# Loading an expert's weights as four serial quarters from one point in time, and one branch per expert slot instead of two

## The chip, the cores and the metric

The kernel runs on one core of one Trainium2 chip. The metric is the device time of one execution in microseconds, as the median of several runs. Engines are named as in the profile: PE (matrix multiply; PEld its weight loads; PEldq its sequencer), DVE, ACT, POOL and SP, which issues most of the DMAs. Three runs of the kernel before gave 836.25 us as the median.

## The reference

Attention with exponential features, then a gated two-layer network, then a mixture of experts. Cut to the last stage, which the change touches:

```python
def _moe2_ref(x, w_gate, w_output_gate, w1, w2):        # x: 2304 x 512, E = 8, F = 1024
    logits = x @ w_gate
    e_idx = np.argmax(logits, axis=1)                   # one expert for each token
    ...
    for e in range(E):
        mask = e_idx == e
        h = np.maximum(x[mask] @ w1[e], 0.0)            # 512 -> 1024
        ye = h @ w2[e]                                  # 1024 -> 512
        out[mask] = gate_w[mask, None] * eom[mask, e, None] * ye
```

## The kernel before

The kernel has three stages one after the other: attention (to about 183 us), the dense network in six blocks of 384 tokens (to about 572 us), and the experts (from 572 us to 824 us). Float32 products are made of three float16 products each: both factors are split into a high and a low part, and low times low is left out (`PARTS`).

In the second stage DVE and ACT also split the weights of all eight experts, and SP stores them in HBM (`split`): for each expert `e` and each matrix `m` (0 is w1, 1 is w2) two halves, the high parts and the low parts, of 1 MB each. So one expert is four pieces of 1 MB.

The third stage works in slots. A slot is up to 128 tokens of one expert, and there are `SLOTS` = 27 of them. The tokens have been scattered by expert into `rows` in HBM. For each slot: POOL gathers 128 rows into `xg` (L668), PE transposes them (L969, 8 matmuls), DVE copies them to `xgt` (L1695), PE multiplies by w1 (`slot_hidden`, L979, 96 matmuls of 128 columns), ACT makes the high part of the ReLU (L1262) and DVE the low part (L1704), PE multiplies by w2 (`slot_output`, L991, 24 matmuls of 512 columns), DVE scales the result (L1714), and POOL scatters it to `out` (L681).

Slots 0 to 2 (`EARLY`) belong to the expert that the first blocks' tokens chose most, "star"; they are written out straight. Slots 3 to 24 are run by a loop of two slots a turn, slots 25 and 26 by the same function `slot` behind it. Which expert a slot has is known only at run time. DVE makes a table of it (L1738 to L1784), `table_ready` tells that it is there, and for every slot PE reads `slot_code` (L1035): whether the slot is used, the parity of its expert's buffer, and `need`, how far the weights must have landed. A slot that isn't used takes two small matmuls (L1054, L1058) instead of the large ones. The program holds the code of both parities, and branches choose between them at run time.

Weights stand in two buffers, `w1_sb[b]` and `w2_sb[b]`, b = 0, 1. Load number k goes into buffer k % 2: k = 0 is the star expert, k = 1 is expert 0, k = 2 is expert 1, and so on to k = 8. All are issued by SP, in the order of its program, with `load_expert(k, e, a, m, half)` at L510; each raises `ew1_loaded` or `ew2_loaded` by 16 when it has landed. A load must wait until the expert that held the buffer before is done with it: `eh_done` counts halves of the first product, `eo_done` second products, and `free_at[e]` is the number of the slot up to which that holds.

On the DMA engines the expert loads (queue q1) meet POOL's gathers and scatters (q0) and fetches of instructions (q8 and q14).

Of the kernel before, what the change touches and what calls it, by code (L numbers as in the profile page):

```python
# [48 lines left out]
EARLY = 3  # L49
# [26 lines left out]
def moe_program(nc, qkt_in, v, w_phi, w_in, w_out, w_gate, w_ogate, w1, w2, out, rows, split, recs):  # L76
# [8 lines left out]
    with ctx:  # L85
# [285 lines left out]
        def _(sp):  # L371
# [133 lines left out]
            def load_expert(k, e, a, m, half):  # L505

                dst, done = ((w1_sb, ew1_loaded), (w2_sb, ew2_loaded))[m]
                if k and not half:
                    sp.wait_ge(done, 32 * k)
                sp.dma_start(dst[a].rearrange("p l c f -> p (l c f)")[:, half * UW:(half + 1) * UW],  # L510
                             split[bass.ds(e, 1), m, :, half * UW:(half + 1) * UW].rearrange("o p n -> (o p) n")).then_inc(done, 16)
# [10 lines left out]
            for half in range(2):  # L522
                load_expert(1, 0, 1, 1, half)
            sp.wait_ge(eh_done, 2 * EARLY)
            for half in range(2):
                load_expert(2, 1, 0, 0, half)
            sp.wait_ge(eo_done, EARLY)
            for half in range(2):
                load_expert(2, 1, 0, 1, half)

            sp.wait_ge(table_ready, 1)
            for e in range(2, E):
                free = sp.value_load(free_at[0:1, e:e + 1], min_val=EARLY, max_val=EARLY + 2 * MAINS)
                sp.wait_ge(eh_done, free * 2)
                for m in range(2):
                    if m == 1:
                        sp.wait_ge(eo_done, free)
                    for half in range(2):
                        load_expert(e + 1, e, (e + 1) % 2, m, half)
# [179 lines left out]
        def _(pe):  # L719
# [311 lines left out]
            slot_transposes(4, 0, 3)  # L1031

            def slot(s, a, turn, more=True):
                p = s - EARLY
# [5 lines left out]
                with pe.If(used):  # L1040
                    with pe.If(parity):
                        slot_hidden(a, 1)
                    with pe.Else():
                        slot_hidden(a, 0)
                    if more:
                        slot_transposes(s + 2, a, turn)
                    pe.wait_ge(ew2_loaded, need)
                    pe.wait_ge(og_ready, s - 1)
                    with pe.If(parity):
                        slot_output(s, a, 1)  # L1050
                    with pe.Else():
                        slot_output(s, a, 0)
                with pe.Else():
# [785 lines left out]
```

## Time and profile before

| | before |
|---|---|
| median of three runs | 836.25 us (835.92 to 836.63) |
| the profiled execution | 836.25 us, span 834.6 us |
| PE busy | 810.8 us, 97% of the span |
| DVE, ACT, POOL busy | 559.7, 387.0, 180.2 us |
| granted TensorE clock, mean | 0.995 |
| share of PE in the chain that ended last | 78% |
| expert loads (L510) | 36 of 1024 KB |

The span goes from the first to the last instruction; 1.65 us of the profiled execution lie outside it. "Busy" of PE means that a matmul is under way. The chain that ended last is followed back from the last instruction, at each step to what released it. For a small change the places count at which PE is idle, and what would make it idle next.

### The profile page before, as it was taken

The numbers are of one execution on the slowest core, as the hardware profiler recorded it, in microseconds if no ns is written. First come the engines' busy times: TensorE is split into PE (matmuls) and PEld (weight loads), VectorE is DVE, ScalarE is ACT, GpSimd is POOL, SyncE is SP. The second block draws the span as 40 slices with busy tenths as digits, with TensorE's granted clock in tenths as the row PEclk, the third lists the DMA queues.
The fourth block names the chain that finished last, engine by engine and source line by source line (L and its number), as shares of the span: only waits on it lengthen the run. The fifth ranks groups of instructions, "written<-read, shape, count | busy, mean of one in ns | idle before, by whom it ended". The sixth has DMA issues, their size and how long they took to land.

```text
span 834.6 us, 19302 instructions
## 1 busy us (share of the span) xinstructions
PE 810.8 (97%) x7110; PEld 509.6 (61%) x7111; DVE 559.7 (67%) x1119; ACT 387.0 (46%) x841; POOL 180.2 (22%) x211
## 2 busy tenths in 40 slices
PE   7999999999999999999999999999899999999995
PEld 5666666665555555555555555556667777777773
DVE  4778888898888888888898897845622543222221
ACT  5777788883654645645646546534101221101110
POOL 4555556761000010010000001010221322111100
PEclk9999999999999999999999999999999999999998
DMA  7466667856665865865764755483173925256500
GB/s 228 136 196 213 203 189 221 222 177 222 221 212 190 223 244 181 258 213 209 220 253 168 252 218 209 122 340 140 60 284 124 392 76 221 91 228 245 233 27 15
DMA packets 67447, 164.36 MB, mean 197 GB/s; under 512 B 28614, under 2 KB 32966, under 8 KB 60736
## 3 DMA queue, kind: packets, MB, share of 16 engines
q1 hardware_dynamic: 61472, 146.74, 51.8%
q0 software_dynamic: 5760, 16.80, 5.6%
q8 instruction: 36, 0.59, 0.3%
q14 instruction: 19, 0.16, 0.1%
q10 hardware_dynamic: 160, 0.07, 0.0%
HBM read 114.16 MB, written 47.55 MB: 194 GB/s over the span
## 4 chain that ended last, share of the span: by engine, by line
PE 78%; DVE 8%; POOL 5%; ACT 4%; issue 3%; another core or an unknown queue 1%; ACTq 0%; DVEq 0%; POOLq 0%
PE ps L894 19%; PE ps L883 17%; PE ps L991 14%; PE ps L979 13%; POOL arena L591 4%; PE ps L771 3%; PE ps L743 3%; PE ps L799 3%; DVE u_mx L1511 2%; ACT arena L1095 2%; PE ps L757 2%; DVE y_words L1503 1%; DVE arena L1536 1%; PE ps L969 1%; PE ps L808 1%
## 5 line engine op out<-in xcount | busy, mean ns | idle before, releaser
L883 PE MATMUL ps<-arena,w_in_sb 128*128 128x384 f16 x1152 | 200.9, 326 | 0.0
L894 PE MATMUL ps<-w_out_sb,arena 128*128 128x512 f16 x576 | 171.3, 379 | 1.3 <-DVE stage L1597 1.3
L883 PEld LDWEIGHTS ps<-arena,w_in_sb 128*128 128x128 f16 x1152 | 111.9, 98 | 81.1 <-issue 0.2
L1262 ACT ACTIVATE x_t<-ps 128x512 f16<-128x512 f32 x54 | 31.6, 596 | 203.8 <-PE ps L979 173.0
L979 PE MATMUL ps<-x_t,arena 128*128 128x128 f16 x2112 | 121.5, 219 | 1.4 <-issue 1.4
L979 PEld LDWEIGHTS ps<-x_t,arena 128*128 128x128 f16 x2112 | 119.2, 98 | 5.3 <-issue 1.8
L991 PE MATMUL ps<-arena,x_t 128*128 128x512 f16 x528 | 119.7, 383 | 2.4 <-DVE x_t L1704 2.4
L894 PE MATMUL ps<-w_out_sb,stage 128*128 128x512 f16 x288 | 109.1, 379 | 0.0
L1234 ACT ACTIVATE arena<-relu 128x384 f16<-128x384 f32 x96 | 50.0, 520 | 119.0 <-DVE relu L1592 119.0
L894 PEld LDWEIGHTS ps<-w_out_sb,arena 128*128 128x128 f16 x576 | 55.7, 98 | 61.5 <-issue 4.5
L1704 DVE SCALAR_TENSOR_TENSOR x_t<-ps,x_t 128x512 f16<-128x512 f32 x54 | 36.7, 689 | 82.4 <-ACT x_t L1262 82.4
L1095 ACT ACTIVATE arena<-ps,arena 128x128 f32<-128x128 f32 x288 | 79.8, 394 | 26.1 <-DVE arena L1287 17.7
L991 PEld LDWEIGHTS ps<-arena,x_t 128*128 128x128 f16 x528 | 51.0, 99 | 60.5 <-ACT x_t L1262 2.8
L1223 ACT ACTIVATE relu<-ps,three,s_h 128x384 f32<-128x384 f32 x96 | 63.4, 661 | 46.3 <-PE ps L883 46.1
L591 POOL TENSOR_TENSOR arena<-arena 128x512 f32<-128x512 f32 (+1 forms) x64 | 69.5, 1085 | 66.5 <-ACT arena L1095 60.8
L1536 DVE SCALAR_TENSOR_TENSOR arena<-arena,u_up 128x1024 f16<-128x1024 f32 x64 | 79.3, 1280 | 4.7 <-ACT arena L1211 4.7
L1211 ACT ACTIVATE arena<-arena,u_up 128x1024 f16<-128x1024 f32 x64 | 72.5, 1140 | 5.6 <-DVE u_up L1528 5.6
L1511 DVE TENSOR_REDUCE u_mx<-arena 128x1 f32<-128x1024 f32 x64 | 74.8, 1211 | 0.0
L641 POOL PARTITION_ALL_REDUCE u_all<-u_red x16 | 7.8, 488 | 301.3 <-DVE u_red L1515 301.3
L1285 DVE TENSOR_REDUCE arena<-ps 128x8 f32<-128x1024 f32 (+1 forms) x48 | 45.9, 957 | 37.2 <-PE ps L743 37.2
L1592 DVE SCALAR_TENSOR_TENSOR relu<-relu,ps 128x384 f32<-128x384 f32 x96 | 52.7, 549 | 25.5 <-ACT relu L1223 24.1
L1714 DVE TENSOR_SCALAR x_t<-ps,stage 128x512 f32<-128x512 f32 x27 | 20.2, 748 | 69.2 <-PE ps L991 69.2
(201 smaller groups left out, 911.8 us busy)
## 6 DMA issues: line engine op xcount, KB each, us to landing
arena<-split SPq DMA_DIRECT2D x36, 1024.0 KB
arena<-in_moe_w SPq DMA_DIRECT2D x16, 2048.0 KB
split<-arena SPq DMA_DIRECT2D x16, 2048.0 KB, 7.4
arena<-in_qkt SPq DMA_DIRECT2D x15, 576.0 KB, 6.5
stage<-in_moe_w_in SPq DMA_DIRECT2D x16, 512.0 KB, 5.0
stage<-in_moe_w_out SPq DMA_DIRECT2D x16, 512.0 KB, 6.2
x_t<-rows POOLq DMA_DIRECT2D x27, 257.0 KB
y_words<-recs SPq DMA_DIRECT2D x32, 144.0 KB, 3.0
```

The source lines that it names most:

```text
L591: nc.gpsimd.tensor_tensor(out, x, y, ALU.add).then_inc(sum_step, 1)
L883: last = nc.tensor.matmul(ps[:, HB[f % GB], 0:BN], w_in_sb[:, lw, c, f * P:(f + 1) * P], xt[:, a, lx, c, :], start=c == 0 and lw + lx == 0 ...
L894: last = nc.tensor.matmul(ps[:, YB + r, :], g_sb[lg_][:, f % GB, r * P:(r + 1) * P], w_out_sb[:, lw, f, :], start=f == 0 and lg_ + lw == 0 ...
L979: last = nc.tensor.matmul(ps[:, bank, f % 4 * P:(f % 4 + 1) * P], w1_sb[b][:, lw, c, f * P:(f + 1) * P], xgt[:, a, lx, c, :], start=c == 0 ...
L991: last = nc.tensor.matmul(ps[:, 6 + a, :], hg[:, a, lh, f, :], w2_sb[b][:, lw, f, :], start=f == 0 and lh + lw == 0, stop=f == EFC - 1 and ...
L1095: last = nc.scalar.activation(pk[:, t0 + t, s, :], ps[:, bank, t * F:(t + 1) * F], ACT.Exp, bias=bias[:, t0 + t:t0 + t + 1], scale=1.0 - 2 ...
L1211: nc.scalar.activation(split_sb[:, 0, q_ * Q:(q_ + 1) * Q], raw[b][:, q_ * Q:(q_ + 1) * Q], ACT.Copy, scale=u_up[:, b:b + 1]).then_inc(u_h ...
L1223: nc.scalar.activation(relu3[:, f % GB, :], ps[:, HB[f % GB], 0:BN], ACT.Relu, bias=three[:, 0:1], scale=s_h[:, 0:1]).then_inc(relu3_ready, 1)
L1234: nc.scalar.mul(g_sb[0][:, f % GB, :], relu3[:, f % GB, :], CG / 6.0).then_inc(g_hi, 1)
L1511: nc.vector.tensor_reduce(u_mx[:, q_:q_ + 1], raw[b][:, q_ * Q:(q_ + 1) * Q], AX.X, ALU.max, apply_absolute_value=True).then_inc(u_searche ...
L1536: nc.vector.scalar_tensor_tensor(out=split_sb[:, 1, cols], in0=raw[b][:, cols], scalar=u_up[:, b:b + 1], in1=split_sb[:, 0, cols], op0=ALU ...
L1592: nc.vector.scalar_tensor_tensor(out=relu3[:, f % GB, :], in0=relu3[:, f % GB, :], scalar=6.0, in1=ps[:, HB[f % GB], 0:BN], op0=ALU.min, o ...
```

## The change

It does two things.

On SP, the four loads of an expert are ordered and gated in another way. Before, w1's two halves went out one behind the other when the first product of the last slot was done (`eh_done`), and w2's two halves when its second product was done (`eo_done`). Now all four wait for `eo_done`, they alternate (w1 high, w2 high, w1 low, w2 low), and each waits until the piece before it of the same matrix has landed. So at most two are under way, one of each matrix. This holds for the star expert and expert 0 too, except that those keep their order of m and half.

On PE, in `slot`, the branch on the parity is taken once instead of twice. The new function `used_slot` holds the first product, the transposes of slot s + 2, the two waits and the second product, and stands once for each parity. The transposes so stand twice in the program.

```diff
             def load_expert(k, e, a, m, half):
                 dst, done = ((w1_sb, ew1_loaded), (w2_sb, ew2_loaded))[m]
-                if k and not half:
-                    sp.wait_ge(done, 32 * k)
+                if k or half:
+                    sp.wait_ge(done, 32 * k + 16 * half)
                 sp.dma_start(dst[a].rearrange("p l c f -> p (l c f)")[:, half * UW:(half + 1) * UW],
...
-            sp.wait_ge(eh_done, 2 * EARLY)
-            for half in range(2):
-                load_expert(2, 1, 0, 0, half)
             sp.wait_ge(eo_done, EARLY)
             for half in range(2):
-                load_expert(2, 1, 0, 1, half)
+                for m in range(2):
+                    load_expert(2, 1, 0, m, half)
...
-                sp.wait_ge(eh_done, free * 2)
-                for m in range(2):
-                    if m == 1:
-                        sp.wait_ge(eo_done, free)
-                    for half in range(2):
+                sp.wait_ge(eo_done, free)
+                for half in range(2):
+                    for m in range(2):
                         load_expert(e + 1, e, (e + 1) % 2, m, half)
...
+            def used_slot(s, a, turn, more, need, b):
+                slot_hidden(a, b)
+                if more:
+                    slot_transposes(s + 2, a, turn)
+                pe.wait_ge(ew2_loaded, need)
+                pe.wait_ge(og_ready, s - 1)
+                slot_output(s, a, b)
...
                 with pe.If(used):
                     with pe.If(parity):
-                        slot_hidden(a, 1)
+                        used_slot(s, a, turn, more, need, 1)
                     with pe.Else():
-                        slot_hidden(a, 0)
-                    if more:
-                        slot_transposes(s + 2, a, turn)
-                    pe.wait_ge(ew2_loaded, need)
-                    pe.wait_ge(og_ready, s - 1)
-                    with pe.If(parity):
-                        slot_output(s, a, 1)
-                    with pe.Else():
-                        slot_output(s, a, 0)
+                        used_slot(s, a, turn, more, need, 0)
```

How SP's program stands at the loads of experts 1 and 2 (k = 2 and 3), before:

```order
L510 DMA arena<-split 128x4096 [waits ew1_loaded,eh_done]
L510 DMA arena<-split 128x4096
L510 DMA arena<-split 128x4096 [waits ew2_loaded,eo_done]
L510 DMA arena<-split 128x4096
L533 TENSOR_LOAD free_at [waits table_ready]
L533 ISA x2
L534 REGISTER_ALU
L510 DMA arena<-split 128x4096 [waits ew1_loaded,eh_done]
L510 DMA arena<-split 128x4096
```

and with the change:

```order
L510 DMA arena<-split 128x4096 [waits ew1_loaded,eo_done]
L510 DMA arena<-split 128x4096 [waits ew2_loaded]
L510 DMA arena<-split 128x4096 [waits ew1_loaded]
L510 DMA arena<-split 128x4096 [waits ew2_loaded]
L531 TENSOR_LOAD free_at [waits table_ready]
L531 ISA x2
L510 DMA arena<-split 128x4096 [waits ew1_loaded,eo_done]
L510 DMA arena<-split 128x4096 [waits ew2_loaded]
```

The wait for `eh_done` is gone, and every load now waits for a landing.

How PE's program stands at slot 3, the first of the loop, from the branch on the parity, before (first both copies of the first product, then the transposes, then the first copy of the second product):

```order
L1041 COMPARE_AND_BRANCH
L979 MATMUL ps<-x_t,arena 128x128 x96
L1041 UNCONDITIONAL_BRANCH
L979 MATMUL ps<-x_t,arena 128x128 x96
L1043 UNCONDITIONAL_BRANCH
L965 ISA
L969 MATMUL ps<-ident,x_t 128x128 [waits xg_loaded1]
L969 MATMUL ps<-ident,x_t 128x128 x7
L1048 REGISTER_ALU [waits ew2_loaded]
L1049 COMPARE_AND_BRANCH [waits og_ready]
L988 REGISTER_ALU
L991 MATMUL ps<-arena,x_t 128x512 [waits hg_ready,hg_hi]
```

and with the change:

```order
L1045 COMPARE_AND_BRANCH
L975 MATMUL ps<-x_t,arena 128x128 x96
L961 ISA
L965 MATMUL ps<-ident,x_t 128x128 [waits xg_loaded1]
L965 MATMUL ps<-ident,x_t 128x128 x7
L1034 REGISTER_ALU [waits ew2_loaded]
L984 REGISTER_ALU [waits og_ready]
L987 MATMUL ps<-arena,x_t 128x512 [waits hg_ready,hg_hi]
L987 MATMUL ps<-arena,x_t 128x512 x11
L984 REGISTER_ALU
L987 MATMUL ps<-arena,x_t 128x512 [waits hg_ready,hg_hi]
L987 MATMUL ps<-arena,x_t 128x512 x11
```

The second copy of the first product, over which the sequencer jumped in the middle of the slot, now stands behind the whole slot with its own transposes and second product, and is jumped over at the slot's end.

## Rows read from the trace of the kernel before

**Rows 1.** The profile's page: part 1, engines' busy time, and part 3, the instruction fetches.

```profile
PE 810.8 (97%) x7110; PEld 509.6 (61%) x7111; DVE 559.7 (67%) x1119; ACT 387.0 (46%) x841; POOL 180.2 (22%) x211
...
q8 instruction: 36, 0.59, 0.3%
```

**Rows 2.** Timeline of PE, 592 to 601 us: start, us, operation, [idle before it <- releaser].

```profile
596.25 4.44 PE L991 MATMUL ps<-arena,x_t 128*128 128x512 f16 x12 [2.36 <-DVE x_t L1704]
```

**Rows 3.** The chain that ended last, 612 to 630 us: start, us, what.

```profile
612.12 5.36 PE ps L979 x96
617.49 0.45 PE ps L969 x8
617.93 5.18 PE ps L991 x24
623.11 1.36 issue
624.47 5.53 PE ps L979 x96
```

**Rows 4.** The same chain, 655 to 666 us.

```profile
658.72 5.42 PE ps L979 x96
```

**Rows 5.** Branches of PE's sequencer at L1049, whole span; then 618 to 624 us alone.

```profile
L1049 PEldq COMPARE_BRANCH  x30: 69/169/3622, 617.0 to 818.0; - x30
...
L1049 PEldq COMPARE_BRANCH  x1: 3622/3622/3622, 619.1 to 619.1; - x1
```

**Rows 6.** L1041, 616 to 618 and 628 to 630 us; L1049, 628 to 633.

```profile
L1041 PEldq COMPARE_BRANCH  x1: 332/332/332, 616.3 to 616.3; - x1
...
L1041 PEldq COMPARE_BRANCH  x1: 306/306/306, 628.9 to 628.9; - x1
...
L1049 PEldq COMPARE_BRANCH  x2: 69/378/687, 629.4 to 631.6; - x2
```

**Rows 7.** The DMA queue of instructions from 620 to 621, then from 629.5 to 630.5 us.

```profile
q8 instruction: 1, 0.02, 5.8%
...
q8 instruction: 1, 0.02, 6.8%
```

**Rows 8.** DMA queues from 634 to 801 us: every queue that moved something.

```profile
q1 hardware_dynamic: 3456, 25.17, 37.9%
q0 software_dynamic: 3120, 8.38, 14.5%
q14 instruction: 2, 0.02, 0.0%
```

**Rows 9.** Windows: us, busy by engine, PEclk, DMA share, GB/s.

```profile
598.00:600.00 2.00, 2.00 (x6) 0.63 (x5) 1.83 (x9) 0.00 (x0) 0.00 (x0) 0.50 0.00 0
...
610.00:612.00 2.00, 2.00 (x17) 1.17 (x16) 0.29 (x2) 0.00 (x0) 0.55 (x1) 1.00 1.04 438
...
618.00:620.00 2.00, 2.00 (x11) 0.94 (x10) 1.48 (x5) 0.12 (x1) 0.00 (x0) 1.00 0.91 334
620.00:622.00 2.00, 2.00 (x11) 0.91 (x10) 0.00 (x0) 0.00 (x0) 0.55 (x1) 1.00 0.42 117
...
624.00:626.00 2.00, 1.53 (x28) 1.54 (x29) 0.02 (x1) 0.00 (x0) 1.02 (x1) 1.00 0.00 0
```

**Rows 10.** SP's loads at L510, first and last start: 611 to 613, then 646 to 650 us.

```profile
L510 SPq DMA_DIRECT2D arena<-split x2: 328/380/433, 611.7 to 612.1; - x2
...
L510 SPq DMA_DIRECT2D arena<-split x2: 328/381/434, 646.6 to 647.0; - x2
```

**Rows 11.** The same line from 541 to 545, then 551 to 553 us.

```profile
L510 SPq DMA_DIRECT2D arena<-split x4: 333/356/711, 541.8 to 543.4; - x4
...
L510 SPq DMA_DIRECT2D arena<-split x2: 338/412/486, 551.8 to 552.2; - x2
```

**Rows 12.** PE's wait for w1 (L1038) at slot 9; POOL's gathers (L668), 650 to 657 us.

```profile
L1038 PEldq ALU_OP  x1: 36/36/36, 657.8 to 657.8; - x1
...
L668 POOL DMA_DIRECT2D x_t<-rows x2: 552/553/554, 650.1 to 655.4; - x2
```

## The prediction

> **What bounds the kernel now.** I read the page first: PE has a matmul under way for 810.8 of 834.6 us [rows 1]. So I looked for the places from 572 us on where PE is idle, since only the expert stage is touched. The timeline and the chain show two. At 593.9 us PE stands 2.36 us for DVE's L1704, and the twelve matmuls behind it take 4.44 us instead of 2.6 [rows 2]. At 623.11 us it stands 1.36 us, released by "issue": PE waits for no engine, its own sequencer is late [rows 3]. Elsewhere up to 824 us a slot is 5.36 (L979) + 0.45 (L969) + 5.18 (L991) = 10.99 us without a gap [rows 3], and no wait of PE for a weight load is among them. The change can therefore save nothing by loading better. It can touch the 1.36 us, and it can open new gaps.
>
> **Why PE stands at 623.11.** The sequencer runs ahead of the matmuls by what is queued: at 619.1 us it has handed out the whole second product of slot 3, which ends at 623.11, so it has 4.0 us in hand. Then its jump at L1049 takes 3.62 us, where the median of 30 such jumps is 0.17 [rows 5]. So slot 4's code is there at 622.7, and behind its register work the first matmul starts at 624.47 [rows 3], 1.75 us later. The sum is 3.62 + 1.75 - 4.0 = 1.4, the gap. During the jump one packet of q8 runs, from 620 to 621 us [rows 7]; q8 moves 0.59 MB in 36 packets, 16 KB each, of instructions [rows 1]. The next such packet that can be told apart is at 629.5 to 630.5 us; behind it a jump at 631.6 takes 0.69 us [rows 6, 7]. From 634 to 801 us there is none at all, so the loop's code is held once it has been passed [rows 8]. The long jump is a first pass over code that has not arrived.
>
> When was that code asked for? I take it that it is asked for when the sequencer enters the piece before it. In the second case that is the jump in the middle of slot 4, at 628.9 us [rows 6]: the packet starts between 629.5 and 630.5, say 1.0 us later, and the code is there at 631.6 + 0.69 = 632.3, 3.4 us after the request. In the first case it is the jump at L1041 at 616.3, which ends at 616.7 [rows 6]. There the packet starts only between 620 and 621 [rows 7], some 3.5 us later and not 1.0: the DMA engines are full until 620 (share 0.91, then 0.42 [rows 9]) with the loads issued at 606 and 611.7 [rows 10]. So the stall is one instruction fetch that stood behind an expert load.
>
> **Part 1, PE's code.** The change takes away the jump in the middle of the slot, 0.33 us in slot 3 [rows 6]. It lies beside the first product, which the sequencer leads by about 1 us, so it is worth nothing, and so in all 22 slots. The transposes stand twice in the program but run once: nothing. What moves is the place of code. Before, the mid-slot jump over a copy of 96 matmuls brought the sequencer at 616.7 into the next piece and asked for the one after it, 2.4 us before the jump at 619.1. Now the sequencer passes 96 + 8 + 24 matmuls in a row and then makes a single jump at the slot's end over a whole slot's copy. The piece with slot 4's code is asked for in the last instructions of the second product or by the jump itself, at 618.9 to 619.1. If nothing were in the way it would be there 3.4 us later, at 622.4, a gain of 0.3. If it waits as long as the one before (3.5 in place of 1.0) it is there at 625.0, a loss of 2.3.
>
> **Part 2, the loads that meet it.** The four loads of expert 1 now start at 611.7 (before: two at 606.1, two at 611.7 [rows 10]). A load of 1 MB at the 438 GB/s of a full window [rows 9] is 2.4 us. Before, 4 MB and the gathers were through by 620. Now 4 MB that start to move at about 613 and share with one gather and one store end near 625. Thus the fetch that is asked for at 619 falls into a full stretch in any case. At most two loads are queued, so I take a wait of about one of them less what has run, 1.3 us rather than the 2.5 seen before. The code is there at 619.0 + 3.4 + 1.3 = 623.7 us, against 622.7. **Term 1: +1.0 us, ends -0.3 and +2.3.**
>
> The Trainium skill's page "Runtime: NRT & Kernel Launch", section "Instruction fetch mechanics", says that prefetch is sequential and that a taken branch out of a window of two pages forces a fetch. By that rule each slot's long jump would cost a fetch; rows 8, with no q8 packet in 167 us of such jumps, speak against it, and it is a rival below. The page "DMA: Bandwidth & Descriptors", section "Queues, rings and completion order", says that a DMA engine takes turns between queues only at the end of a packet. The late packet of rows 7 agrees; it gives no other sum.
>
> **Part 3, later weights.** Loads of w1 start one second product (5.6 us) later than before, and every piece waits for the last one of its matrix. Each expert with two slots or more hides that: its loads have 22 us. The tight place is expert 2, since expert 1 has only slot 7 (647 to 658). Its w1 loads were issued at 641.0 and are now due at 646.6 [rows 10]. PE asks for them at slot 9, at 657.8 [rows 12], and with an unused slot in front it has next to nothing in hand there: its first matmul of slot 9 starts at 658.72 [rows 4], 0.9 us later, and the register work alone takes most of that. So 11.2 us are left for w1 low, the third of four MB. The nearest row: at 541.8 four loads were issued together, and w1's second, the third MB, had landed at 551.8, 10.0 us later [rows 11]. That is 656.6. Two gathers (650.1 and 655.4 [rows 12]) and one store of 256 KB, 0.6 us each, share the engines: +0.6 to +1.8, so 657.2 to 658.4. The serial issue adds nothing as long as w2 high is still moving when w1 low is issued, and it moves for 2.4 us while an issue takes about 1.1. **Term 2: +0.1 us, ends 0 and +1.0.** w2 is needed 5.5 us later and lands at about 660.5: nothing. Behind these loads SP has only the next expert's to issue, and they all start from `eo_done`.
>
> **Part 4, the first loads.** Star and expert 0 now go out piece by piece from 541.8. Star, issued at 541.8 and landed some 12 us later, is needed at 572; expert 0's last two loads, which wait for the end of the dense stage at 572 as before, are needed behind slot 3's first product, at 617.9 [rows 3]. A few us more are hidden in both. The gathers of slots 0 and 1 are issued at 563 behind the scattered rows, which share with fewer loads than before: nothing.
>
> **The sum** is made against the profiled execution, 836.25 us, which is also the median: 836.25 + 1.0 + 0.1 = 837.35, say 837.4 us.
>
> **The rivals.**
> 1. The fetch finds a gap between two loads, or the shorter burst before 619 leaves it free. Then term 1 is 0 or negative, to the whole 1.36 at most: 834.9 to 836.2. For it: only two loads are queued instead of four. Against it: 4 MB from 613 on can't be over by 619. Chance 0.2.
> 2. The gap at 623 grows past 2 us and PE's clock falls. Rows 2 show it: behind the 2.36 us gap twelve matmuls took 4.44 instead of 2.6, 1.85 us lost, at a granted clock of 0.50, the 1.2 GHz level; behind the 1.36 us gap it stayed at 1.00 [rows 2, 9]. Term 1 is then +1.2 to +2.3 and +1.85 comes on top: 839.3 to 840.5. It decides from a gap of about 2 us. Against it: my middle value for the gap is 2.4 us, just at that edge, and the half of the cases below it stays clear. Chance 0.15, slower.
> 3. w1 of expert 2 lands late, beyond 657.8 by 0.5 to 1.5 us; in sum 838 to 839. Chance 0.15.
> 4. Faster: the gap of 2.36 us at 593.9 and its 1.85 us of slow clock shrink, since ACT, on which DVE waits there, was released by nothing that the profile names. If that is a fetch of ACT's that meets other traffic now, up to 4.2 us go: 832 to 834.5. Nothing that the change moves runs at 590. Chance 0.05.
> 5. By the rule of the Runtime page each of about 20 used slots pays its long jump: 20 gaps of 1.4 us, 864 us. Chance 0.01.
>
> **How the numbers follow.** The forecast's case has 0.44, from 836.0 to 838.7. 0.2% is about what a measurement of this kernel can tell from no change: 1.67 us, the limits are 834.6 and 837.9. Faster holds rival 4 and a little of rival 1: 0.07. Slower holds rivals 2, 3 and 5 and a quarter of the forecast's case: 0.40. The rest, 0.53, is the same. The range from 835.4 to 840.2 leaves out rival 4, the fast end of rival 1 and the last of rival 2.
>
> **What would show it.** The gap before slot 4, 1.36 us now, is 2 to 3 us, with a q8 packet inside the sequencer's long jump, which now stands at the end of slot 3. No gap at slot 9, and SP's third load of expert 2 is issued near 651.5. The mid-slot jump is gone and the slots still take 10.99 us. The prediction is wrong if the gap at 623 vanishes or stays as it is, if PE waits for weights at any other slot, or if PE's gap at 593.9 has changed.

## The result and the profile after

The kernel after took 840.96 us as the median of six runs (839.78 to 843.92), the kernel before 835.48 us beside it (833.18 to 836.63). The ratio is 1.0055, with a 95% interval from 1.0032 to 1.0079: slower by 2.7 to 6.6 us. The record holds 31 more executions of the kernel after: over all 37 the median is 839.78 us (835.77 to 844.21). The forecast was 837.4 us with a range up to 840.2. The median of the 37 lies inside it and that of the six 0.8 us outside. The sign was right, but the forecast called a change within 0.2% the likeliest, and its added time of 1.1 us is a quarter to a fifth of what was measured.

The profiled execution of the kernel after took 835.77 us, span 834.1 us, which is the lowest of the 37. So its rows are read for gaps, and its total is not taken for the kernel's. The page, where rows 1 stood:

```profile
PE 807.9 (97%) x7110; PEld 508.1 (61%) x7111; DVE 559.6 (67%) x1119; ACT 387.0 (46%) x841; POOL 180.1 (22%) x211
...
q8 instruction: 36, 0.59, 0.3%
```

The work is the same, and so is the number of code packets (36). The timeline of PE at the two places where before stood [rows 2, 3], first 588 to 600 us, then 612 to 636:

```profile
590.69 5.34 PE L987 MATMUL ps<-arena,x_t 128*128 128x512 f16 x24
...
621.92 5.53 PE L975 MATMUL ps<-x_t,arena 128*128 128x128 f16 x96 [3.47 <-issue]
...
634.57 1.62 PE L975 MATMUL ps<-x_t,arena 128*128 128x128 f16 x26 [1.49 <-issue]
```

At 593 us there is no gap in this execution: 24 matmuls of L987 (L991 before) run in one piece at full clock. Where before stood 1.36 us ahead of slot 4, PE now stands 3.47 us, and 1.49 us ahead of slot 5, where it did not stand at all before. The chain that ended last shows the third place, slot 9:

```profile
612.96 7.11 DMA arena<-split
620.08 1.85 issue
621.92 5.53 PE ps L975 x96
...
633.08 1.49 issue
...
657.82 0.36 issue
658.18 5.53 PE ps L975 x96
```

The matmuls themselves take what they took in rows 3. The chain puts the first gap down to a weight load that lands at 620.07 us. That is no more than the last semaphore event ahead of the gap; slot 4 uses expert 0, whose weights had long landed, and the experiments come back to it. What PE's sequencer did is in its branches at L1045, the single parity jump of a slot (whole span, then 612 to 618, then 628 to 632 us; ns min/median/max, and when):

```profile
L1045 PEldq COMPARE_BRANCH  x30: 63/177/5773, 606.6 to 811.2; - x30
...
L1045 PEldq COMPARE_BRANCH  x1: 5773/5773/5773, 614.4 to 614.4; - x1
...
L1045 PEldq COMPARE_BRANCH  x1: 3289/3289/3289, 629.0 to 629.0; - x1
```

Two jumps are long, and the median of 30 is 0.18 us. The first starts at 614.42 and ends at 620.19; the first matmul follows 1.73 us later, at 621.92. Slot 3's second product ends at 618.45, so the sequencer had 4.03 us in hand: 5.77 + 1.73 - 4.03 = 3.47, the gap. The code packets of q8 lie inside both jumps, at 617.81 and at 630.02 us (the windows 617 to 618 and 630 to 631):

```profile
q8 instruction: 1, 0.02, 5.8%
...
q8 instruction: 1, 0.02, 6.0%
```

The DMA engines round them (us, busy by engine, PEclk, DMA share, GB/s):

```profile
616.00:618.00 2.00, 2.00 (x11) 0.89 (x10) 0.00 (x0) 0.00 (x0) 0.14 (x1) 1.00 0.99 412
618.00:620.00 2.00, 0.45 (x3) 0.00 (x0) 0.75 (x1) 0.00 (x0) 0.00 (x0) 1.00 1.02 345
620.00:622.00 2.00, 0.08 (x2) 0.09 (x3) 0.00 (x0) 0.00 (x0) 1.02 (x1) 1.00 0.90 328
622.00:624.00 2.00, 2.00 (x38) 2.00 (x39) 0.00 (x0) 0.00 (x0) 0.00 (x0) 1.00 0.56 225
...
628.00:630.00 2.00, 2.00 (x11) 0.93 (x10) 1.48 (x5) 0.09 (x1) 0.00 (x0) 1.00 0.00 0
```

The first jump starts in full traffic, and the packet comes 3.4 us after the jump's start. The second starts in a window with no traffic, and the packet comes after 0.97 us. In both cases the jump ends 2.3 to 2.4 us after the packet's start. Ahead of slot 5 the sequencer also needs more than the 1.73 us: it first closes the loop's turn, which makes 2.23 us from the jump's end at 632.34, and 3.29 + 2.23 - 4.03 = 1.49, the second gap. The burst of weight loads now lasts longer. Against the end of slot 3's second product the last packet of q1 ended 0.8 us ahead before (622.3 against 623.11) and ends 5.9 us behind it now (624.3 against 618.45). SP's loads (L510) of the expert 1, its last two, and of the expert 2, its last two, then SP's wait for w1 of the expert 2 (L509), where rows 10 stood:

```profile
L510 SPq DMA_DIRECT2D arena<-split x2: 328/328/328, 613.0 to 617.2; - x2
...
L510 SPq DMA_DIRECT2D arena<-split x2: 327/328/328, 650.8 to 654.3; - x2
...
L509 SPq EVENT_SEMAPHORE  x1: 17/17/17, 657.4 to 657.4; - x1
```

**The account.** Against the profiled execution of before: +2.11 at slot 4 (3.47 against 1.36), +1.49 at slot 5, +0.36 at slot 9, together +3.96 us, 0.47%. In the other direction the stop at 593.9 and its slow clock are absent, 2.36 and 1.85 us [rows 2], which are 4.21 of the 4.66 us by which slot 3 ends sooner (618.45 against 623.11 [rows 3]): 834.6 + 3.96 - 4.66 is 833.9, and the span is 834.1. (Times of the two traces can therefore only be compared against a slot's own.) The stop at 593 is not the change's doing, as the runs below show, so the change by itself costs about 4 us in this trace, within the interval of the timed runs.

### The profile page after: what moved, and what is told of

It reads as the page before. It is cut to its first block, busy times and chain, and to the rows that moved or that the text cites. A ratio compares the mean times of both kernels' runs of the same rounds, so it can differ in the third digit from the quotient of the medians.

```text
span 834.1 us, 19259 instructions
## 1 busy us (share of the span) xinstructions
PE 807.9 (97%) x7110; PEld 508.1 (61%) x7111; DVE 559.6 (67%) x1119; ACT 387.0 (46%) x841; POOL 180.1 (22%) x211
## 4 chain that ended last, share of the span: by engine, by line
PE 76%; DVE 8%; POOL 5%; ACT 4%; issue 4%; DMA 2%; ACTq 0%; DVEq 0%; POOLq 0%
PE ps L890 19%; PE ps L879 17%; PE ps L987 13%; PE ps L975 13%; POOL arena L587 4%; PE ps L767 3%; PE ps L739 3%; PE ps L795 3%; DVE u_mx L1507 2%; ACT arena L1091 2%; DMA arena<-split 2%; PE ps L753 2%; DVE y_words L1499 1%; DVE arena L1532 1%; PE ps L804 1%
## 5 line engine op out<-in xcount | busy, mean ns | idle before, releaser
L987 PE MATMUL ps<-arena,x_t 128*128 128x512 f16 x528 | 117.9, 379 | 0.0
L1700 DVE SCALAR_TENSOR_TENSOR x_t<-ps,x_t 128x512 f16<-128x512 f32 x54 | 36.7, 689 | 82.4 <-ACT x_t L1258 82.4
L987 PEld LDWEIGHTS ps<-arena,x_t 128*128 128x128 f16 x528 | 50.5, 98 | 56.8
```

Source lines behind the costliest of these rows:

```text
L987: last = nc.tensor.matmul(ps[:, 6 + a, :], hg[:, a, lh, f, :], w2_sb[b][:, lw, f, :], start=f == 0 and lh + lw == 0, stop=f == EFC - 1 and ...
```

## The experiments

Each was timed in rounds against the kernel before on the same chip. The gaps are those of PE in one profiled execution of each. The kernel before itself was profiled only once, so its gap of 1.36 us is taken over to the other chips; the kernels with its branches and with the loads of the change, profiled on two of them, had 1.34 and 1.25 us there. One theory stands behind most of them. **Theory A:** PE's code comes in pieces of 16 KB; a piece is asked for when the sequencer enters the one before it; and a request that falls into a burst of weight loads comes late. The rivals are that the slot waits for weights, that the single branch costs by itself, and that the new waits of SP cost by themselves.

### Each half of the change alone

**One branch alone.** Before's loads, and PE's program as changed:

```diff
                     with pe.If(parity):
-                        slot_hidden(a, 1)
+                        used_slot(s, a, turn, more, need, 1)
                     with pe.Else():
-                        slot_hidden(a, 0)
-                    ...
+                        used_slot(s, a, turn, more, need, 0)
```

> The change's PE part alone (one branch per slot, used_slot); SP loads as before. Theory A (the loss is the code's: code is asked for only when the sequencer gets to the piece before it, and one jump at the slot's end asks too late): both gaps of the changed kernel stay, before slot 4 (1.4 to 3.5 us, by how much of the load burst is left at 618 us) and before slot 5 (about 1.5 us); no gap at slot 9; time +1.5 to +3.6 us over before. Theory B (the loss is the loads': later, serial loads): one gap of 1.36 us before slot 4 as before, none before slot 5, time as before within 0.5 us.

Measured: 833.67 us against 831.82, ratio 1.0016 [1.0003, 1.0029]. Its chain from 614 to 641 us:

```profile
619.96 2.34 issue
622.30 5.53 PE ps L979 x96
...
633.45 1.99 issue
635.44 5.53 PE ps L979 x96
```

The jumps ahead of both gaps took 4.59 and 3.78 us, and 0.46 us more stood at 670.19. The first jump's packet came after 1.80 us, though the DMA engines were as full (share 0.99 and 0.94) as in the kernel after, where it took 3.39. This profiled execution was the slowest of its twelve runs (836.79 us, 3.1 above the median), so its gaps are larger than the usual ones. The branch part costs 0.3 to 2.4 us by the timed runs.

**The loads alone.** Before's two branches, and SP's program as changed:

```diff
-                if k and not half:
-                    sp.wait_ge(done, 32 * k)
+                if k or half:
+                    sp.wait_ge(done, 32 * k + 16 * half)
...
-            sp.wait_ge(eh_done, 2 * EARLY)
-            ...
             sp.wait_ge(eo_done, EARLY)
             for half in range(2):
-                load_expert(2, 1, 0, 1, half)
+                for m in range(2):
+                    load_expert(2, 1, 0, m, half)
```

> The change's SP part alone (all four loads from eo_done, alternating, each behind the landing of the one before it); PE code as before. Theory A: no gap before slot 5; before slot 4 a gap of 0 to 1.5 us, since the code is asked for at 616.7 as before and meets another part of the burst; at slot 9 a gap of 0.3 to 0.4 us (w1 low of expert 2 landed at 657.4 in the changed kernel); time within 1 us of before. Theory B: the whole loss of the changed kernel, +4 to +5 us.

Measured: 832.08 us against 831.82, ratio 1.0003 [0.9995, 1.0012]. PE stands 1.34 us ahead of slot 4, as before did, and 0.66 us ahead of slot 9, where the chain says:

```profile
653.61 0.66 issue
654.27 5.53 PE ps L975 x96
```

w1 of the expert 2 landed at 653.5, and the first matmul followed 0.77 us later, the slot's register work. So the halves cost 0.16% and 0.03%, and together 0.55% (0.52% on the next chip). By the medians most of the loss is neither one's own. The intervals allow less: the upper ends of the halves add up to 0.41%, the lower ends of the whole are 0.32 and 0.33%. What the traces show of it is where they meet: the branch moves the request for code to the end of a slot, and the loads of the change stretch the burst over that moment. The branch alone already opens both gaps; the loads lengthen the first one, from 2.34 us even in this slow execution to 3.47.

### The change again, on another chip

No edit.

> The changed kernel as it is, on the chip of this call, so that the others of the call can be held against it, and for a second look at its gaps. Theory A (fetch of code): the gaps before slots 4 and 5 are there again, the first between 1.4 and 3.5 us by how the fetch meets the loads, the second about 1.5 to 2 us; a gap of 0.3 to 0.7 us at slot 9; time +0.3 to +0.6% over before.

Measured: 839.68 us against 834.84, ratio 1.0052 [1.0033, 1.0071]. PE stood 2.40 us at 593.14, 3.45 at 620.71, 0.62 at slot 9 and 0.31 at 672.21, and not at slot 5. The jump took 5.69 us, from 616.75. The windows behind it (us, busy by engine, PEclk, DMA share, GB/s), and under them two pieces of the chain:

```profile
622.00:624.00 2.00, 0.00 (x0) 0.00 (x0) 0.00 (x0) 0.00 (x0) 1.02 (x1) 1.00 0.79 324
624.00:626.00 2.00, 1.84 (x29) 1.85 (x30) 0.00 (x0) 0.00 (x0) 0.00 (x0) 0.87 0.38 141
626.00:628.00 2.00, 2.00 (x22) 2.00 (x20) 0.00 (x0) 0.00 (x0) 0.00 (x0) 0.50 0.00 0
628.00:630.00 2.00, 2.00 (x31) 2.00 (x30) 0.69 (x1) 0.60 (x1) 0.00 (x0) 0.78 0.00 0
```

```profile
622.26 1.90 issue
624.16 7.15 PE ps L975 x96
```

Behind the gap the granted clock fell to 0.50, the 1.2 GHz level, and slot 4's first product took 7.15 us in place of 5.53. That is rival 2 of the prediction. The account here: 3.45 - 1.36 + 1.62 + 0.62 + 0.31 = +4.6 us, 0.56% against the measured 0.52%. The two executions of one program lose about the same (4.0 and 4.6 us) in different ways: one by a second gap, the other by the clock.

### Is it the moment of the request, or the traffic?

**The change with the expert 1's loads one slot later.**

```diff
-            sp.wait_ge(eo_done, EARLY)
+            sp.wait_ge(eo_done, EARLY + 1)
```

> The changed kernel with the four loads of expert 1 issued one slot later (eo_done of slot 3 in place of slot 2; with these inputs expert 0 has slots 3 to 5, so they are in time), so that the DMA engines are free while the jump at the end of slot 3 waits for code, and full while the jump at the end of slot 4 does. Theory A: the jump at slot 3's end takes about 3.3 us in place of 5.8 and the gap before slot 4 shrinks from 3.5 to about 1.1 us; the gap before slot 5 grows from 1.5 to 2 to 4 us. If the burst has nothing to do with it (the gaps are the jump's own): 3.5 and 1.5 us as in the changed kernel.

Measured: 834.31 us against 831.82, ratio 1.0037 [1.0024, 1.0050]. Gaps: 1.42 ahead of slot 4, 2.46 ahead of slot 5, 0.38 at slot 9. The first jump, at 613.77, found no traffic: its packet started 1.00 us later and the gap fell from 3.47 to 1.42. But the loads now ran beneath the next request: the jump of 4.19 us at 626.34 got its packet only after 1.87 us.

```profile
L1045 PEldq COMPARE_BRANCH  x3: 63/3713/4192, 613.8 to 626.3; - x3
```

Moving the traffic moves the loss with it: 1.42 - 1.36 + 2.46 + 0.38 = +2.9 us, 0.35%. A gap of 1.4 us stays even with free DMA engines, because the request comes no earlier than the jump: a packet after 1.0 and its code 2.7 us later make 3.7, and 3.7 + 1.7 - 4.0 is 1.4. The branch part therefore costs even without traffic, as long as the limit of a piece falls there.

**The kernel before with w2 of the expert 1 held back by one first product** (some 5.6 us, until that of slot 3 is done). Here the traffic is thinned at the moment of before's own request:

```diff
+            sp.wait_ge(eh_done, 2 * EARLY + 2)
             sp.wait_ge(eo_done, EARLY)
```

> The kernel before, with the two w2 loads of expert 1 held back from 611.7 until slot 3's first product is done (eh_done 8, about 617.3 us). The fetch of slot 4's code, asked for at 616.7, then finds the engines free. Theory A: the jump L1049 at 619.1 takes about 1.0 us in place of 3.6, the gap of 1.36 us before slot 4 is gone, and the time falls by 1.3 us (0.16%). If the stall is the jump's own and not the burst's: the gap stays 1.4 us and the time as before.

Measured: 828.64 us against 831.82, ratio 0.9968 [0.9949, 0.9986]. The gap ahead of slot 4 is gone (below, slot 3's second product and slot 4's first in the chain), and PE stands nowhere else in the expert stage:

```profile
611.40 5.18 PE ps L992 x24
616.58 5.36 PE ps L980 x96
```

and the jump at L1050 that took 3.62 us in before takes 1.06:

```profile
L1050 PEldq COMPARE_BRANCH  x1: 1057/1057/1057, 612.5 to 612.5; - x1
```

The request went out with the mid-slot jump at 609.8, and its packet started at 611.15, 1.35 us later instead of 4.0. This is the strongest support for theory A: PE's program is untouched, nothing that slot 4 needs has moved, and its gap goes. It was run again on a third chip:

> The kernel before with the second matrix of the expert 1 held back by one slot, run again on this chip. The theory expects the gap of before at 623 us (1.36 us) gone and a ratio of 0.995 to 0.999 again. If the first measurement (0.9968) was an accident of its chip, the ratio is 0.9995 to 1.001 and a gap of over 1 us stands somewhere between 600 and 640 us.

Measured: 832.98 us against 834.12, ratio 0.9982 [0.9969, 0.9996]. The gap ahead of slot 4 is gone again (the jump took 1.22 us), and 1.03 us stands elsewhere, at 667.91. It is faster than before in both measurements, by 0.04 to 0.5%; more can't be said of the size. The expected 0.16% lies at the near end of the first interval and within the second.

### Is it the place of the code?

**The change with 80 instructions more ahead of the slots.** They are waits that have long been met, spread behind the first products of the last dense block. They shift the code of the slots and do nothing else:

```diff
+                    if not more:
+                        for _pad in range(10):
+                            pe.wait_ge(consts_made, 2)
```

(The number 80 counts instructions as built; two waits stand in one, so each place holds five and not the ten of the source.)

> The changed kernel with 80 more instructions in PE's program ahead of the slots (waits on a semaphore that has long been reached, five behind each first product of the last dense block, where they cost the sequencer some 0.25 us each and PE nothing), and nothing else. Theory A (code comes in pieces of 16 KB, and the next piece is asked for when the sequencer gets into one): the limits of the pieces now fall 80 instructions earlier in a slot's code. The one in slot 3 is passed before the second product's first half and not after the slot, about 2 us earlier: the gap before slot 4 falls to 0 to 1.5 us. The one in slot 4 is passed in the first product: the gap before slot 5 is gone. Time falls by 2 to 4 us against the changed kernel. If the long jump itself is what costs (Theory C), both gaps and the time stay.

Measured: 834.31 us against 834.84, ratio 0.9996 [0.9982, 1.0010], on the chip on which the change itself had 1.0052. Its chain at slot 4 and at slot 9:

```profile
615.11 5.40 DMA arena<-split
620.50 0.69 issue
621.20 5.53 PE ps L978 x96
...
655.31 0.58 issue
```

PE stands 0.97 us ahead of slot 4 in place of 3.45, and not at all ahead of slot 5. The packet started 0.79 us behind the jump's start in place of 3.3, and the traffic was no thinner (us, busy by engine, PEclk, DMA share, GB/s):

```profile
616.00:618.00 2.00, 2.00 (x11) 0.94 (x10) 0.74 (x4) 0.00 (x0) 0.55 (x1) 1.00 1.04 408
```

So the request must have gone out well ahead of the jump; the trace doesn't show when. No loss is left that the measurement can tell, with the loads and the branches of the change untouched. It also settles the rival that the chain suggests. If slot 4 waited for the weight load that the chain names, its first matmul would follow the landing at a fixed distance. It follows it by 1.85 us (after), 1.90 (again), 0.69 (here), 0.64 (loads alone) and 0.07 (without the waits, below). To the end of the long jump the distance is 1.7 to 1.8 us in all of them, and in before [rows 3, 5].

**The kernel before with 160 instructions more.** The same edit with 20 waits.

> The kernel before, with 160 instructions more of waits that are long met in TensorE's program ahead of the slots (spread over the last dense block, 10 behind each first product), so that the limits between the pieces of its code lie 160 instructions earlier in the slots; nothing else moves. The theory (which piece is asked for when decides the gap) expects the gap of 1.36 us ahead of the slot 4 to change: gone or below 0.5 us if the next piece is now asked for ahead of the burst at 612 to 621 us, 2 to 4 us in another slot if within it, so a ratio of 0.997 to 1.004 with the gap's change equal to the time's. The rival (the gap belongs to the data that the slot waits for, or to the long jump as such) expects the gap to stay at 1.0 to 1.8 us ahead of the slot 4 and the ratio at 0.9995 to 1.0015.

Measured: 835.31 us against 834.12, ratio 1.0008 [0.9989, 1.0026]. The chain:

```profile
617.86 1.98 issue
619.85 0.62 PE ps L972 x8
```

The gap has left the place ahead of slot 4 (I had expected it gone or in another slot). It stands now inside slot 3, between the first product and the transposes, where the mid-slot jump takes 2.96 us, and it is 0.6 us larger than the 1.36 of before. The rival (the gap belongs to the slot, and stays) is out. The time moved by no more than the measurement's error, which fits 0.6 us but doesn't prove it.

**The two parity copies swapped**, with one branch and before's loads:

```diff
+                other = pe.snap((code // 2 + 1) % 2)
-                    with pe.If(parity):
-                        used_slot(s, a, turn, more, need, 1)
+                    with pe.If(other):
+                        used_slot(s, a, turn, more, need, 0)
                     with pe.Else():
-                        used_slot(s, a, turn, more, need, 0)
+                        used_slot(s, a, turn, more, need, 1)
```

> One branch per slot and loads as before, but the copy for buffer 0 stands first. Slots 3 to 5 have buffer 1, so now they jump over a copy at their start, and fall through at the end. Theory A: no gap before slot 5; the code lacks early in slot 3 instead (the piece behind the jump's target is asked for only 1 us ahead, in a full burst): one gap of 2 to 5 us in or before slot 3's first product, and one of 1 to 3 us before slot 4. Theory C (a jump at the slot's end costs): no gaps at all but the 1.36 us of before.

Measured: 838.58 us against 834.84, ratio 1.0037 [1.0023, 1.0050]. The chain:

```profile
609.85 3.38 issue
613.23 8.35 PE ps L979 x96
```

Of the two gaps that theory A expected, the first is there: 3.38 us ahead of slot 3's first product, at 609.85, behind a jump of 4.16 us, and half clock from 612.35 to 619.17 made that product 8.35 us. The second, ahead of slot 4, is not, and none stands ahead of slot 5; 0.68 us more stood at 672.66. So my count of where the limits lie places some gaps and not others. Theory C, which expected nothing but the old 1.36 us, is out: the order of two equal copies moves the gap.

### Do SP's waits cost?

**Order and start of the change, without the waits for landing**, with before's branches:

```diff
-                if k or half:
-                    sp.wait_ge(done, 32 * k + 16 * half)
+                if k and not half:
+                    sp.wait_ge(done, 32 * k)
```

> The SP part alone, without the added waits of the low halves for the landing of the high halves: all four loads of an expert still go out together at eo_done, w1 and w2 in turn. PE code as before. If slot 9's gap (0.66 us with the waits) comes from the later start alone, it stays 0.4 to 0.7 us; if the serial issue has a part in it, w1 low lands up to 1.5 us earlier and the gap is gone. The gap before slot 4 stays between 0 and 1.5 us. Time as with the waits, within 0.7 us.

Measured: 835.42 us against 834.84, ratio 1.0013 [0.9996, 1.0030]. PE stands 1.25 us at slot 4, 1.48 at slot 9 and 1.04 at 667.92. The chain at slot 4, then at slot 9:

```profile
609.45 11.16 DMA arena<-split
620.61 0.07 issue
620.68 5.53 PE ps L975 x96
...
655.15 0.69 DVE x_t L1700
655.85 0.44 issue
656.28 5.53 PE ps L975 x96
```

With four loads under way together w1 isn't earlier: it took 12.1 us from the first issue, and 11.8 with the waits. The waits for landing cost nothing that shows, and the gap at slot 9 comes from starting w1 one second product later (the run below with the old starting points hasn't got it). That this gap is larger here, 1.48 against 0.66, isn't explained: the chain names DVE's L1700, and PE's sequencer passed its wait for w1 at 655.5, 0.6 us after SP had passed its own for the same semaphore.

**Before's starting points, with the waits for landing and the expert 1's w2 held back.**

```diff
-                if k and not half:
-                    sp.wait_ge(done, 32 * k)
+                if k or half:
+                    sp.wait_ge(done, 32 * k + 16 * half)
...
+            sp.wait_ge(eh_done, 2 * EARLY + 2)
             sp.wait_ge(eo_done, EARLY)
```

> TensorE's program is that of before, with its two parity branches for each slot. SyncE asks for the experts' weights at before's points (w1 when the hidden products of the expert ahead are done, w2 when its outputs are), but waits with each second half until the first has landed, as the change does, and the second matrix of the expert 1 is held back by one slot, as in the run that beat the kernel before. The theory (a piece of TensorE's code that is asked for while weight loads keep the DMA engines busy comes late) expects no gap in the expert stage over 0.5 us and a ratio of 0.996 to 0.998. The rival, that the delay of the loads pays by itself by way of the second halves' waits and not by the free moment for the code, expects the waits to show as a gap of 0.3 to 1.5 us ahead of the slot 9 and a ratio of 0.998 to 1.000.

Measured: 832.98 us against 834.12, ratio 0.9987 [0.9974, 1.0001]. One gap of 0.61 us, ahead of slot 5, and none at slot 4 or 9:

```profile
631.44 0.61 issue
```

With w1 asked for at the old point the gap at slot 9 is gone, as part 3 of the prediction has it. The theory's two figures were narrowly missed (no gap over 0.5 us, a ratio of at most 0.998), and the rival's gap at slot 9 isn't there; its range for the ratio holds the measured one. Against the same kernel without the waits (0.9982, same chip) they make no difference that shows.

### Is the single branch worth anything?

The kernel just shown, with the single branch and the 80 instructions:

```diff
+                    if not more:
+                        for _pad in range(10):
+                            pe.wait_ge(consts_made, 2)
...
-                        slot_hidden(a, 1)
+                        used_slot(s, a, turn, more, need, 1)
```

> The loads as in the run with the old points and the waits on the first halves, and TensorE's program as changed, with one branch for each slot and the 80 instructions more ahead of the slots that took the gap away. What is asked is whether the single branch is worth anything by itself once no code comes late. The theory of the prediction (the second branch costs 0.0 us, since the sequencer runs ahead of the products) expects the same time as the run with before's branches within 0.1% and slots 10.99 us apart. The rival (each branch costs) expects 0.2 to 0.5 us for each of the 21 slots, so 4 us or more less than that run, a ratio of 0.992 or below.

Measured: 833.19 us against 834.12, ratio 0.9989 [0.9976, 1.0002]; the two branches gave 0.9987 on the same chip. From slot 3 on PE has no gap at all in its profile (0.76 us at 604.94, ahead of the slots, where the chain waits for the gather of rows). So with no code late the branch that is taken away is worth nothing that shows over the 19 slots that take it; each ratio is known to 0.13%, and the rival's 4 us or more (0.5%) are out. The chain at the step from slot 3 to slot 4, with nothing between:

```profile
615.16 5.18 PE ps L995 x24
620.35 5.36 PE ps L983 x96
```

## Why the prediction was right and wrong

- **What bounds the kernel, and what can't be gained:** right. The slots are as long as before, PE waited for no weight load in the expert stage before, and the branch taken away gains nothing that shows once no code is late.
- **Why PE stands at 623.11 in before** (a code fetch asked for at 616.3 that stood behind an expert load): right, and now shown. With the loads thinned at that moment the fetch started after 1.35 us and the gap went. With the code shifted it moved. The prediction overlooked one packet there. It called the packet of 629.5 to 630.5 the next behind the one at 620, but there is one between them, in the window 623.5 to 624.5 (shown below the list). It starts at 623.97, 1.3 us after the long jump's end at 622.71, which fits the rule that was assumed (entering a piece asks for the next) and changes no term.
- **Part 1, the request moves to the slot's end:** right. The packet started inside the single long jump.
- **Term 1, +1.0 us with ends -0.3 and +2.3:** the mechanism was right and the size too low. I took a wait of about one load less what has run, 1.3 us above the free case. Measured, the packet started 3.4 us after the jump's start against 0.97 in free traffic, 2.4 more, so the gap grew by 2.11, near the far end. The reason I gave for the small value (at most two loads are queued, not four) doesn't hold: with two loads under way the DMA share was 0.99 and 1.02 in the windows round the packet. Full engines don't fix the size either. With before's four loads and the single branch the packet came after 1.80 us at a share of 0.99 and 0.94. What sets the wait within a burst stays open.
- **The second gap:** missed. I followed the request for slot 4's code and left the one for slot 5's at its old lead, though I had just read it in rows 6 and 7. The mid-slot jump of slot 4 asked for it at 628.9 in before, and its code was there in time for the jump at 631.6. Without that jump the request comes with the one at the slot's end, here at 629.05, and even with free engines 3.29 us of jump and 2.23 us of register work are more than the lead of 4.03: 1.49 us. The sum of the prediction had no term for it. The argument of part 1 had to be made at each first pass over a piece, and I made it at one. It is +1.49 in one execution and 0 in the other, where the clock fell instead.
- **Term 2, +0.1 with ends 0 and +1.0:** the mechanism was right and the size low. Slot 9's gap is 0.36 and 0.62 us. w1 landed at 657.4, 11.7 us after the expert's first load was issued (645.75), where 10.6 to 11.8 had been worked out. SP's third load went out 5.1 us after the first (I had 4.9). Slot 9's first matmul followed the landing by 0.78 us, 0.36 us after it was due.
- **That the serial issue adds nothing:** right; without the waits w1 landed no sooner.
- **Rival 1, term 1 at 0 or below:** out; the gap grew in both executions.
- **Part 4, the first loads:** right. No gap between 572 and 590 us that before hadn't.
- **Rival 2, the clock:** seen, behind 3.45 us in one execution of two, for +1.62 us. I gave it 0.15 with a limit of about 2 us for the gap. My own middle value for the gap, 2.4 us, was as long as the one in rows 2 behind which the clock had fallen, so it belonged into the likeliest case.
- **Rival 4:** the gap at 593.9 was absent in the profile after, and I had said that this would prove me wrong. It didn't follow from the change. The same program had it on another chip (2.40 us); it was absent in all four kernels of one chip, two with before's branches, and present in all eight of two other chips, at 2.33 to 2.40 us. It goes by the chip or the execution, and a comparison of two single traces would have booked 4.2 us of it as a gain.
- **The signs of being wrong that I had named:** two came, PE's wait at slot 9 and the changed gap at 593.9, and the gap ahead of slot 4 was 3.5 us and not the 2 to 3 expected. That the median of all 37 executions lies in the range, at its slow end, is in part luck: the range was spread for the clock and for late weights, and no term stood in it for slot 5.
- **Rival 5, a fetch for each long jump:** out. From 634 us on the jumps took 0.2 us, 0.34 at most, and q8 moved 36 packets as before, none of them between 633.1 and 801.4 us. The Trainium skill's page "Runtime: NRT & Kernel Launch", section "Instruction fetch mechanics", says that fetching runs ahead sequentially and that a taken branch out of a window of two pages forces a fetch. For the first pass the trace agrees with the first half of it; for the loop's later turns it speaks against the second half, since neither the jumps at 15 used slots over a whole copy nor the loop's jumps back over two slots' code, which had taken four packets (617.81 to 633.10), fetched anything.

The packet between, in before's window 623.5 to 624.5:

```profile
q8 instruction: 1, 0.02, 6.0%
```

The sum, put right by the rows: 836.25 + 2.1 + 1.5 (or 1.6 of slow clock) + 0.4 to 0.9 = 840.3 to 840.9 us. That is 4.0 to 4.6 us above before, against the measured 0.55% or 4.6 us (2.7 to 6.6), and against medians of 840.96 (six executions) and 839.78 (all 37).

**What stays open.** Why the request for slot 5's code led its jump in the one execution of the change (jump at 632.91, packet already at 632.08) and not in the other (629.05, 630.02). What the gaps of 0.3 to 1.0 us around 668 to 672 us wait for, which some executions have and some don't. What makes the wait for a packet in a burst anything from 1.8 to 4.0 us. What ACT waits for ahead of the stop at 593 us: it stands 5.5 us there in before, released by nothing that the profile names, and 2.1 us in after, which has no stop. And exactly which instruction of a piece sends the request: the run with swapped copies shows that my count doesn't place it.

## What to carry to other kernels

A loop body that is passed for the first time while the DMA queues are full pays for its code: look in the trace for long branches of the sequencer with an instruction packet inside them, and lay the data burst beside such moments, not over them. Here one wait of SP that held back 2 MB for about one product gained 0.2 to 0.3% by the medians, and no change of branches gained anything. An edit that only moves code can shift the time by 0.5% through where the pieces' limits fall (1.0052 to 0.9996 here), so test a structural change of a large unrolled program with some padding ahead of it before you judge it; a pair of changes also has to be costed together where one sets when something is asked for and the other what it meets.

## What the runs showed of the hardware

- **A piece of PE's code, from request to use.** From the packet's start to the end of the jump that waited for it: 2.3 to 2.8 us in all 25 cases of the 14 traces. From the jump taken to have asked to the packet's start: 0.97 to 1.06 us in seven cases with free DMA engines (share 0.00 in between), 1.1 to 1.6 us in three with a share of 0.13 to 0.53, and 1.8 to 4.0 us in ten with 0.8 or more. (The padded kernels, in which no jump asks, are left out.)
- **The clock behind one and the same gap.** Behind the gap of 2.33 to 2.40 us at 593 us the granted clock fell to 0.50 in four executions (among them before) and stayed at 1.00 in five. Behind 3.47 us ahead of slot 4 it stayed, behind 3.45 us it fell. A fall that lasts 3.4 us costs 1.6 to 1.9 us. A limit like the 2 us of the prediction's rival 2 decides nothing here.
- **Padding is cheap.** 80 instructions of long-met waits in PE's program, spread over the dense block, took no time that shows: the kernel with them and the single branch (0.9989) and the one without them and with two branches (0.9987) are 0.02% apart, each known to 0.13%.
